# Clustered attention with two expert layers: the first expert's row numbers, a wider table of fillers, and one sum for the numbers

## The reference

```
x = attention per head, where a query and a key see each other only if both
    have the same nearest of 16 centroids          # B 2, H 8, S 768, D 64
x = x.reshape(1536, 512)

# first expert layer: 8 experts of 192 rows each
logits = x @ w_gate                                # 1536 x 8
for idx in argsort(-logits.flatten()):             # the largest first
    tok, e = idx // 8, idx % 8
    if assigned[tok] >= 0 or counts[e] >= 192: continue
    assigned[tok] = e; counts[e] += 1
out[mask_e] = relu(x[mask_e] @ w1[e]) @ w2[e]      # 512 -> 1024 -> 512

# second expert layer: 4 experts, every row through each
p = domain_probs / (domain_probs.sum(-1) + 1e-9)
out += p[:, e] * (relu(x @ v1[e]) @ v2[e])
```

## Time and profile before

| | |
|---|---|
| three runs | 1019.0, 1019.85, 1020.62 us, median 1019.85 |
| profiled execution | 1019.42 us, span 1017.6 us |
| PE busy | 999.1 us, 98% of the span |
| DVE / ACT / POOL busy | 611.8 / 444.6 / 425.4 us |
| mean granted TensorE clock | 0.995 |
| chosen stretch of the search | 296.5 to 473 us, PE busy nearly throughout |

### The profile page before, as it was taken

One profiled execution on the slowest core, in us unless ns is written; L12 is line 12 of the kernel. 1 busy time (PEld: TensorE's weight loads), 2 busy tenths in 40 slices (PEclk: granted clock), 3 DMA queues, 4 the chain that ended last, 5 costly groups with the idle time before them and its releaser, 6 DMA issues.

```text
span 1017.6 us, 18267 instructions
## 1 busy us (share of the span) xinstructions
PE 999.1 (98%) x6642; PEld 921.0 (91%) x6642; DVE 611.8 (60%) x1355; ACT 444.6 (44%) x862; POOL 425.4 (42%) x349
## 2 busy tenths in 40 slices
PE   8999999999999999999999999999999999999997
PEld 7889999999988999999999889999889998889995
DVE  6888888888867455556045445554486554455543
ACT  5888888888830111113342333322343323223320
POOL 5233233332201111112456757556567765566542
PEclk8999999999999999999999999999999999999999
DMA  5232323223155555556722122122112321221201
GB/s 159 56 78 67 86 73 85 77 81 82 31 126 182 183 182 181 182 182 205 249 75 83 42 83 72 53 84 67 57 63 83 125 83 45 80 83 51 74 1 63
DMA packets 87314, 99.63 MB, mean 98 GB/s; under 512 B 18097, under 2 KB 57041, under 8 KB 87249
## 3 DMA queue, kind: packets, MB, share of 16 engines
q1 hardware_dynamic: 84960, 92.38, 30.0%
q0 software_dynamic: 2288, 6.36, 1.9%
HBM read 79.81 MB, written 6.32 MB: 85 GB/s over the span
## 4 chain that ended last, share of the span: by engine, by line
PE 93%; DVE 3%; ACT 1%; POOL 1%; issue 1%; DMA 0%; DVEq 0%; POOLq 0%
PE ps_y L1569 10%; PE ps_y L1568 10%; PE ps_y L1567 10%; PE ps_h L1594 8%; PE ps_y L1609 8%; PE ps_h L1569 7%; PE ps_h L1567 7%; PE ps_h L1568 7%; PE ps_t L1448 6%; PE ps_s L1435 4%; PE ps_o L1462 3%; PE ps_o L1463 3%; PE ps_s L1436 3%; PE ps_m L1482 2%; PE ps_m L1409 2%; PE ps_m L1395 1%
## 5 line engine op out<-in xcount | busy, mean ns | idle before, releaser
L623 POOL TENSOR_TENSOR w_lo<-w_sum,w_hi 128x1792 fp32r<-128x1792 f32 x32 | 129.9, 4083 | 62.4 <-ACT w_hi L829 62.4
L1569 PE MATMUL ps_y<-b_lo,h_hi 128*128 128x512 f32 x384 | 149.7, 390 | 0.0
L1568 PE MATMUL ps_y<-b_hi,h_lo 128*128 128x512 f32 x384 | 149.7, 390 | 0.0
L1567 PE MATMUL ps_y<-b_hi,h_hi 128*128 128x512 f32 x384 | 149.4, 389 | 0.0
L1357 DVE SCALAR_TENSOR_TENSOR Y<-ps_y,ids_all,Y 128x512 f32<-128x512 f32 x84 | 63.0, 750 | 134.9 <-PE ps_y L1569 134.9
L1567 PE MATMUL ps_h<-x_hi,w_hi 128*128 128x384 f32 x384 | 128.6, 335 | 0.0
L1569 PE MATMUL ps_h<-x_lo,w_hi 128*128 128x384 f32 x384 | 128.5, 335 | 0.0
L1568 PE MATMUL ps_h<-x_hi,w_lo 128*128 128x384 f32 x384 | 128.4, 334 | 0.0
L629 POOL TENSOR_TENSOR b_lo<-b_raw,b_hi 128x2048 fp32r<-128x2048 f32 x16 | 74.0, 4622 | 116.2 <-ACT b_hi L836 115.4
L1008 DVE TENSOR_TENSOR p_lo<-ps_t,p_hi 128x384 fp32r<-128x384 f32 x192 | 99.9, 548 | 26.7 <-ACT p_hi L749 25.2
L999 DVE TENSOR_REDUCE neg_max<-ps_s 128x1 f32<-128x768 f32 x96 | 91.3, 951 | 14.8 <-PE ps_s L1436 14.3
(11 more groups left out here) (241 smaller groups left out, 2221.6 us busy)
## 6 DMA issues: line engine op xcount, KB each, us to landing
w_sum<-in_moe_w_dram SPq DMA_DIRECT2D x64, 256.0 KB, 3.2
b_raw<-in_moe_w_dram SPq DMA_DIRECT2D x16, 1024.0 KB, 5.2
raw_a<-in_moe_w_dram SPq DMA_DIRECT2D x8, 1024.0 KB
raw_b<-in_moe_w_dram SPq DMA_DIRECT2D x8, 1024.0 KB, 8.4
odd_a<-in_moe_w_dram SPq DMA_DIRECT2D x8, 1024.0 KB
odd_b<-in_moe_w_dram SPq DMA_DIRECT2D x8, 1024.0 KB, 8.3
khhT<-kqT SPq DMA_DIRECT2D x32, 192.0 KB, 3.1
raw_k<-in_k_dram SPq DMA_DIRECT2D x16, 192.0 KB, 2.4
```

What stands on the lines that cost most here:

```text
L623: g.tensor_tensor(w_lo[t][:], w_sum[t][:, 1:8], w_hi[t][:].bitcast(F32), ALU.subtract).then_inc(wlo_done[t], 1)
L1567: t_.matmul(dst, w_hi, x_hi, start=first, stop=False)
L1568: t_.matmul(dst, w_lo, x_hi, start=False, stop=False)
L1569: return t_.matmul(dst, w_hi, x_lo, start=False, stop=last)
```

## The change

- `F_FIRST`, the fillers of phase 1: the entries between count and digit of steps 2, 3 and 4 go from 1 to 2, the entry ahead of the ranks from 5 to 6. That is 21 products in place of 17. The other tables stay, so each later place in PE's order finds the stream of products four further on.
- In phase 0 the three closing operations stand behind the numbers instead of ahead of the ranks; in later phases they stay.
- `place` gets three columns whose sum is the row number (4, 2 and the remainder), so one reduction takes the place of the copy and the multiply-add. L1652's matmuls write 15 columns in place of 14, and POOL makes one more small pattern at the start.
- ACT copies the turned rows in two pieces, and the hidden products wait for the piece that they read.

```diff
-    F_FIRST = (0,) * 4 + (3, 1, 3, 1, 3, 1, 5, 0)
+    F_FIRST = (0,) * 4 + (3, 2, 3, 2, 3, 2, 6, 0)
...
-        place = sb("place", [P, NT, 2 + 3 * E2], BF16)
+        place = sb("place", [P, NT, 3 + 3 * E2], BF16)
...
-            for i, (pattern, mult) in enumerate((([[P, B], [0, TPB]], 1), ([[0, B], [1, TPB]], 0))):
+            for i, (pattern, mult) in enumerate((([[4 * P, B], [0, TPB]], 4), ([[2 * P, B], [0, TPB]], 2),
+                                                   ([[0, B], [1, TPB]], 0))):
...
                 act.wait_ge(xt_full, m + 1)
-                s.copy(xe[:].rearrange("p (a c) m -> p a c m", a=2), xe_ps).then_inc(xe_done, 1)
+                for a in range(2):
+                    s.copy(xe[:, 2 * a:2 * a + 2, :], xe_ps[:, a]).then_inc(xe_done, 1)
...
                 dve.wait_ge(ids_full, n + 2)
                 at = ps_tok[0:HS, 0:2 * W].rearrange("p (s a) -> p s a", s=2)
-                link(v_.tensor_copy(place_lo[0:HS, :], at[:, :, 1]))
-                v_.scalar_tensor_tensor(out=ids[0:HS, n, :, 0], in0=at[:, :, 0], scalar=float(TPB),
-                                        in1=place_lo[0:HS, :], op0=ALU.mult, op1=ALU.add).then_inc(ids_ready, 1)
+                with nc.allow_low_precision(reason="whole numbers under 2 ** 24"):
+                    v_.tensor_reduce(ids[0:HS, n, :, 0], at[:, :, 0:3], AX.X, ALU.add).then_inc(ids_ready, 1)
...
+                def close_chosen():
+
+                    add(v_.tensor_scalar(closing[:], e_b[:], e_top[:], GONE, ALU.is_equal, ALU.mult))
+                    link(v_.tensor_tensor(e_sum[:], e_sum[:], e_top[:], ALU.add))
+                    link(v_.tensor_tensor(logit[:], logit[:], spread(closing[:], 1, shape), ALU.add))
+
                 v_.tensor_scalar(e_num[:, n:n + 1], e_top[:], -1.0, float(E), ALU.mult,
                                  ALU.add).then_inc(e_chosen, 1)
-                add(v_.tensor_scalar(closing[:], e_b[:], e_top[:], GONE, ALU.is_equal, ALU.mult))
-                link(v_.tensor_tensor(e_sum[:], e_sum[:], e_top[:], ALU.add))
-                link(v_.tensor_tensor(logit[:], logit[:], spread(closing[:], 1, shape), ALU.add))
+                if n > 0:
+                    close_chosen()
                 take_slots(n)
                 slots_hot(n)
                 if n == 0:
                     for s in range(2):
                         first_token_ids(s)
+                    close_chosen()
...
-                if st == 0:
-                    pe.wait_ge(xe_done, m + 1)
+                if st < KD and st % 2 == 0:
+                    pe.wait_ge(xe_done, 2 * m + st // 2 + 1)
```

More of the change, by code:

```diff
@@ L503, in _ @@
                    allow_small_or_imprecise_dtypes=True).then_inc(const_ready, 1)
-            for i, (pattern, mult) in enumerate((([[P, B], [0, TPB]], 1), ([[0, B], [1, TPB]], 0))):
+            for i, (pattern, mult) in enumerate((([[4 * P, B], [0, TPB]], 4), ([[2 * P, B], [0, TPB]], 2),
+                                                   ([[0, B], [1, TPB]], 0))):
                 g.iota(place_f[:, :, i], pattern, base=0, channel_multiplier=mult,
                        allow_small_or_imprecise_dtypes=True).then_inc(const_ready, 1)
-            pool.wait_ge(const_ready, 9)
-            g.tensor_copy(place[:, :, 0:2], place_f[:]).then_inc(const_ready, 1)
+            pool.wait_ge(const_ready, 10)
+            g.tensor_copy(place[:, :, 0:3], place_f[:]).then_inc(const_ready, 1)
             def search_constants():
@@ L946, in _ @@
                              ALU.mult).then_inc(cen_rows, 1)
-            dve.wait_ge(const_ready, 10)
+            dve.wait_ge(const_ready, 11)
             dve.wait_ge(zeros_done, 2)
@@ L1070, in _ @@
             mlink(v_.tensor_tensor(mix_n[:], mix[:], spread(mix_s[:], 2, [P, NT, E2]), ALU.mult), 4)
[L1071 to L1074, removed]
+            mlink(v_.tensor_copy(place[:, :, 3:3 + E2], mix_n[:]), 5)
+            mlink(v_.tensor_tensor(mix[:], mix_n[:], place[:, :, 3:3 + E2], ALU.subtract), 6)
+            mlink(v_.tensor_copy(place[:, :, 3 + E2:3 + 2 * E2], mix[:]), 7)
+            mlink(v_.tensor_tensor(place[:, :, 3 + 2 * E2:], mix[:], place[:, :, 3 + E2:3 + 2 * E2],
                                    ALU.subtract), 8)
@@ L1147, in slots_hot @@
                                      spread(slot[:, n % 2], 2, hot), ALU.is_equal).then_inc(hot_ready, 1)
-            W = 2 + 3 * E2
+            W = 3 + 3 * E2
             def token_ids(n):
@@ L1164, in first_token_ids @@
                 at = (ps_tok, ps_tok_0)[s]
-                link(v_.tensor_copy(place_lo[0:HS, s:s + 1], at[0:HS, 1:2]))
-                v_.scalar_tensor_tensor(out=ids[0:HS, 0, s, 0:1], in0=at[0:HS, 0:1], scalar=float(TPB),
-                                        in1=place_lo[0:HS, s:s + 1], op0=ALU.mult, op1=ALU.add).then_inc(ids_ready, 1)
+                with nc.allow_low_precision(reason="whole numbers under 2 ** 24"):
+                    v_.tensor_reduce(ids[0:HS, 0, s, 0:1], at[0:HS, 0:3], AX.X, ALU.add).then_inc(ids_ready, 1)
             def first_token_mix():
@@ L1190, in token_mix @@
                 at = ps_tok[0:HS, 0:2 * W].rearrange("p (s a) -> p s a", s=2)
-                link(v_.tensor_copy(mix_lo[0:HS], at[:, :, 2 + 2 * E2:]))
-                link(v_.tensor_tensor(mix_mid[0:HS], mix_lo[0:HS], at[:, :, 2 + E2:2 + 2 * E2], ALU.add))
-                v_.tensor_tensor(ids[0:HS, n, :, 1:].bitcast(F32), mix_mid[0:HS], at[:, :, 2:2 + E2],
+                link(v_.tensor_copy(mix_lo[0:HS], at[:, :, 3 + 2 * E2:]))
+                link(v_.tensor_tensor(mix_mid[0:HS], mix_lo[0:HS], at[:, :, 3 + E2:3 + 2 * E2], ALU.add))
+                v_.tensor_tensor(ids[0:HS, n, :, 1:].bitcast(F32), mix_mid[0:HS], at[:, :, 3:3 + E2],
                                  ALU.add).then_inc(mix_ready, 1)
```

9 lines of the change are left out of this document (4 added, 5 removed).

## The result

| | us |
|---|---|
| before, median of 6 runs | 1020.21 (1019.0 to 1021.15) |
| after, median of 6 runs | **1025.24** (1023.33 to 1026.21) |
| ratio after / before | 1.0049, 95% interval 1.0040 to 1.0059 |
| profiled execution of after | 1025.16 |

The change makes the kernel 0.5% slower, 5.0 us between the medians. The profile after, first lines of the page: the span, and the shares of the chain that ended last, which answer to the earlier trace rows.

The account below looks back on a forecast made before the run. PE, with 93% of the chain, was taken to bound the kernel. Phase 1's -0.6 us and +5.9 of waiting made +5.3: profiled 1019.42 becomes 1024.7, and with the median 0.4 above, 1025.1 us, range 1022.8 to 1027.0.

Parts of the forecast that it names:

- The waiting, +5.9 us: Phases 3 to 6 and behind them: PE waits for gathered rows in five places, +5.9 us, bounds 4.5 and 6.5.
- All of the 1.3 us becomes waiting: Phase 4, repeated in phase 6: PE already waited at the transposes, so the whole 1.3 us lead turns into waiting.
- the landing keeps its distance to them within 0.05 us: Gathered rows land a fixed time behind the A loads (10.6 us phase 3, 10.65 phase 4); sooner numbers save 0.25 us.
- The rival, that it follows the gather: Rows land as much sooner as the gather is issued, 5 x 0.17 = 0.85 us; waiting 5.3; chance 0.23.
- the queues taking turns: DMA engines alternate between queues, so A's load shares with the gather; result +4.7, 1024.5 us; chance 0.23.
- Phase 1 and the start: Start of the search and phase 1: +0.31 - 0.1 + 0.5 - 1.3 = -0.6 us.
- 3 x 0.15: Phase 1, steps 2 to 4: a second product between count and digit makes each step 0.15 us longer.
- PE's 36 fillers hold the 24 matmuls: Phase 0: uncut fillers run to 313.26, so moving the closing operations gains nothing for the numbers' first half.
- The two products don't fit: Rival, phase 1: a second product delays each digit by its whole 0.325 us; result +6.0, 1025.9 us; chance 0.13.
- The rows are there when PE comes: Rival: the gather lands 1.3 us sooner, 9.3 behind A; waits vanish, 1019.2 us; chance 0.05, partial form 0.06.
- The clock: Rival: TensorE's clock falls after each of five waits, 2.5 us more each, +17.8 in all, 1037.6 us; chance 0.03.
- My argument from the row around 51 us: Against the clock falling: PE was busy for 0.02 of a whole microsecond there, and the clock stayed at 1.00.

Follow-up runs that it names:

- e1: The changed kernel with the old F_FIRST table and the other three edits kept: +0.1 us against the kernel before, ratio 0.9997.
- e2: The kernel before with only the new F_FIRST table: +5.2 us against the kernel before, ratio 1.0050.
- e3: The changed kernel with four products fewer in phase 2's last stretch (11 to 7): -0.1 us against the kernel before, ratio 0.9998.
- e5: The changed kernel with the second half of matrix load A issued only when the expert's gathered rows have landed: +3.7 us against the kernel before, ratio 1.0034.
- e6: The changed kernel with three linked DVE operations ahead of the numbers in phases 2 to 6, 0.57 us later: +7.1 us against the kernel before, ratio 1.0075.
- e11: The changed kernel with nine linked DVE operations ahead of the numbers, 1.7 us later: +22.8 us against the kernel before, ratio 1.0207.
- e7: The changed kernel with the edits of e3 and e5 together: -0.6 us against the kernel before, ratio 0.9994.
- e10: The kernel before with A's second half behind the gathered rows, except for the expert loaded in phase 6: +0.1 us against the kernel before, ratio 0.9998.
- e12: e9 with the closing operations back in their old place ahead of the ranks' multiply: -1.7 us against the kernel before, ratio 0.9982.
- e4: The changed kernel with the numbers one place sooner on DVE, ahead of picking the next digit, in phases 2 to 6: +5.9 us against the kernel before, ratio 1.0055.
- e9: e7 with the expert of phase 6 loaded as before, both halves at once: -1.2 us against the kernel before, ratio 0.9984.
- e8: The kernel before with only e5's edit, A's second half behind the gathered rows: -0.5 us against the kernel before, ratio 0.9994.

## Why the prediction was right, and where it was not

- **The mechanism** was the forecast's: transposes tied to a stream that is four products ahead, five waits for the gathered rows, none given back. e1 and e2 put the whole loss on the table, e3 on the lead.
- **The waiting, +5.9 us, was too much: 4.88.** Per place I had 0.9, 1.3, 0.85, 1.3 and 1.8; the stages grew by 0.79, 0.71, 0.78, 0.77 and 1.83 (55.11 - 54.58 + 1.30). The step that failed is "All of the 1.3 us becomes waiting" in phases 4 and 6. I took one landing of before as the time at which rows land in that phase. Phase 4's and phase 6's were late ones (4.01 and 3.84 us behind g2, where the changed kernel has 3.58 and 3.49), and the first digits ahead of those transposes were late by 0.12 and 0.15 us, against 0.01 and 0.06 in the changed kernel. Counted from undisturbed phases the changed kernel waits 4.37 + 1.83 = 6.2 us, but the kernel before had lost 1.3 of its own, 0.9 of that by late digits.
- **What the landing hangs on** was wrong. I read "the landing keeps its distance to them within 0.05 us" out of two phases. The same trace has 10.26 us in phase 5 and 10.15 in phase 2, so "the shortest here being 10.6" was wrong too, and in the changed kernel the distances to A lie between 9.96 and 10.52. The rival, that it follows the gather, was no better as a rule: with the whole of A ahead, B came 3.2 to 4.55 us behind g2. The reading of e5's expectation, the later of 10.1 us behind A and 3.3 behind g2, holds in its second half only. Where A's stream is over as g2 starts, B came 3.2 to 3.5 us behind g2 in phases 3 to 6 (phases 3 and 5 of the kernel before, phase 3 of the changed one, e6, and e11 but for one of 4.37), and in e5, e7 to e10 and e12 the second half of A, issued on the same landing, came 3.2 to 3.4 behind; where A runs on, B came 3.35 to 4.55 behind. How much later doesn't follow from how long A runs on. The half microseconds from g2's start (the last number is GB/s), in phase 4 of e3, where B came 3.35 behind, and of the kernel before, where it came 4.01 behind:

```profile
392.67:393.17 0.50, 0.50 (x5) 0.50 (x4) 0.00 (x0) 0.00 (x0) 0.50 (x1) 1.00 1.05 389
393.17:393.67 0.50, 0.50 (x7) 0.43 (x6) 0.00 (x0) 0.00 (x0) 0.50 (x2) 1.00 1.07 361
```
```profile
390.90:391.40 0.50, 0.50 (x5) 0.50 (x4) 0.00 (x0) 0.00 (x0) 0.49 (x1) 1.00 1.02 377
391.40:391.90 0.50, 0.50 (x12) 0.44 (x11) 0.00 (x0) 0.00 (x0) 0.50 (x2) 1.00 0.96 258
```

That, the exception in e11, and the place behind phase 6, which is nearly always later (3.8 us or more), are open. Of the queues taking turns, which the Trainium skill has in DMA: Bandwidth & Descriptors, section Queues, rings and completion order, the runs show only that a gather beside the end of a load often lands later; no row shows the turns themselves.
- **Phase 1 and the start**, forecast -0.6 us: phase 1 took 19.12 us in place of 18.32 for 1.30 us more of products, and phase 2 is equal, so -0.50. The 0.80 us are 0.21 up to the first count (0.31 in the forecast), -0.08 between the second and the third, where the turned rows come in (-0.1), 0.16 and 0.14 for two steps, 0.33 for the last step's digit, and 0.04 from there to the ranks. So the term "3 x 0.15" measured 0.63: I had taken it for three equal steps, and the last one had no room for a second product. "PE's 36 fillers hold the 24 matmuls" was wrong: those had waited for `slot_hot`, and start 2.07 us behind the ranks in place of 2.25, so DVE came to the search sooner too.
- **"The two products don't fit"** fell in two of the three steps (count to digit 1.04 us) and held in the last one, 0.18 us above the forecast's 0.15.
- **"The rows are there when PE comes"** fell: with the whole of A ahead no landing came sooner than 9.8 us behind A (e3), and 9.3 was needed.
- **The clock** didn't fall in the changed kernel. My argument from the row around 51 us held for every wait up to 1.84 us, and failed for the five from 1.95 us on (e4, e11), and the price that I gave, 2.5 us a fall, was about right (1.7 to 2.9).
- **The median** came out 0.1 us from the forecast by luck, because errors met: 0.9 us too much for the change (5.3 for 4.4), against a kernel before that ran 0.4 us longer beside it (1020.21 for 1019.85) and a distance of the medians that is 0.6 us more than the stages explain.

## What to carry to other kernels

More filler work in one stretch moves every later instruction that is tied to the same stream: look for what it waits for there, and take the lead back where nothing waits (e3), before counting the gain. A load that is issued ahead of a small, urgent gather can delay it, here by up to 1.2 us; put what isn't needed yet behind the gather (e5), but see whether something at the end waits for the queue (e7, e9). Before a wait in one profile is taken as a phase's own, compare it with the same place in the other phases, and look whether what stands ahead of it came late for another reason (e8, e10).

## What the hardware showed beyond that

- Waits of TensorE for the rows of 0.2 to 1.84 us (the changed kernel, e1, e2, e3, e5, e6, and the rest of e4 and e11) left the granted clock at 1.00 in the 5 us behind each; waits of 1.95, 2.06, 2.08, 2.32 and 3.19 us were each followed by 0.66 or 0.50.
- A gather instruction of POOL took 1.57 us in place of 0.97 beside DVE's `reach`, in each place of e4 where they met.
- A gather with free DMA engines landed 3.2 to 3.4 us behind g2 in phases 3 to 6 of e5 to e10 and e12. With the end of a load beside it, it was 3.35 to 4.55.
- In phases 3 to 6 of the kernel before, the changed one, e1, e2, e3, e9, e10 and e12, DVE took up the first count 1.5 to 1.6 us behind its own last operation, though the count was done by then. In e4 to e8 it took it up as the count ended. The cause is open.
